# Attention stage of a three-part kernel: another order of the steps within a turn

## What is computed

```python
# q, k, v: 4 x 8 x 576 x 64; mean over 4 neighbouring positions gives q_d, k_d, v_d (144 positions)
out_d = sm_attn(q_d, k_d, v_d)                 # pooled branch: softmax over all 144
out_up = np.repeat(out_d, factor, axis=2)
mask = np.abs(pos[:, None] - pos[None, :]) < factor
scores = np.where(mask, scale * np.matmul(q, k.transpose(0, 1, 3, 2)), -1000000000.0)
out_local = np.matmul(softmax(scores), v)      # local branch: 7 neighbours
x = (out_up + out_local)                       # -> 2304 x 512
h = x @ w_in; x = (h * np.tanh(softplus(h))) @ w_out            # 512 -> 2048 -> 512
...                                            # second block: 512 -> 1024 -> 512
```

## Time and profile before

| | us |
|---|---|
| median of 3 runs (707.36 to 709.15) | 707.73 |
| the profiled execution | 707.11 |
| its span, first to last instruction | 705.3 |
| TensorE busy | 678.3 (96%) |
| VectorE busy | 369.9 (52%) |
| ScalarE busy | 262.5 (37%) |
| GpSimd busy | 183.2 (26%) |

### The profile page before, as it was taken

One profiled execution on the slowest core, in us unless ns is written; L12 is line 12 of the kernel. 1 busy time (PEld: TensorE's weight loads), 2 busy tenths in 40 slices (PEclk: granted clock), 3 DMA queues, 4 the chain that ended last, 5 costly groups with the idle time before them and its releaser, 6 DMA issues.

```text
span 705.3 us, 12609 instructions
## 1 busy us (share of the span) xinstructions
PE 678.3 (96%) x5098; PEld 626.7 (89%) x5098; DVE 369.9 (52%) x675; ACT 262.5 (37%) x583; POOL 183.2 (26%) x220
## 2 busy tenths in 40 slices
PE   5878799999999999999999999999999999999998
PEld 5667689999999999999999999999778888888886
DVE  8999966642223222322232332664796667756671
ACT  5788874321112111211121112136564444535441
POOL 5989820000000000000000000574535434354100
PEclk9999999999999999999999999999999999999999
DMA  7887783000000000000000030002000000000001
GB/s 239 234 236 221 209 309 147 1 1 0 1 1 1 1 0 1 1 1 1 0 2 1 1 119 1 1 1 90 31 16 16 30 31 16 16 31 30 31 16 45
DMA packets 25657, 37.51 MB, mean 53 GB/s; under 512 B 2944, under 2 KB 13184, under 8 KB 25472
## 3 DMA queue, kind: packets, MB, share of 16 engines
q1 hardware_dynamic: 25600, 36.72, 16.3%
HBM read 31.99 MB, written 4.72 MB: 52 GB/s over the span
## 4 chain that ended last, share of the span: by engine, by line
PE 82%; DVE 10%; issue 3%; ACT 2%; POOL 2%; DMA 1%; SPq 0%; DVEq 0%; ACTq 0%; POOLq 0%
PE psum L685 28%; PE psum L671 28%; PE psum L778 12%; PE psum L755 11%; PE psum L764 2%; DVE prob L1110 2%; DVE mx L1107 1%; DVE xy L1134 1%; ACT pprob L839 1%; DVE den L1124 1%; DVE psum L1098 1%; POOL ylo L548 1%; DMA qkT<-kT_dram 1%; DVE so L1296 1%; DVE kd L1073 1%
## 5 line engine op out<-in xcount | busy, mean ns | idle before, releaser
L1193 DVE CAST ghi<-g_sb 128x384 fp32r<-128x384 f32 x96 | 39.6, 413 | 245.5 <-PE psum L685 188.8
L894 ACT ACTIVATE g_sb<-psum 128x384 f32<-128x384 f32 x96 | 47.0, 490 | 292.6 <-PE psum L671 288.3
L671 PE MATMUL psum<-xhi,whi 128*128 128x384 f32 x384 | 129.7, 338 | 1.3 <-ACT g_sb L894 0.7
L671 PE MATMUL psum<-xlo,whi 128*128 128x384 f32 x384 | 129.1, 336 | 0.0
L685 PE MATMUL psum<-ghi,whi 128*128 128x384 f32 x384 | 129.1, 336 | 0.0
L685 PE MATMUL psum<-ghi,wlo 128*128 128x384 f32 x384 | 129.1, 336 | 0.0
L671 PE MATMUL psum<-xhi,wlo 128*128 128x384 f32 x384 | 129.1, 336 | 0.0
L685 PE MATMUL psum<-glo,whi 128*128 128x384 f32 x384 | 129.1, 336 | 0.0
L520 POOL TENSOR_TENSOR t<-raw 128x1024 f32<-128x1024 f32 x1 | 2.6, 2609 | 350.3 <-PE psum L685 350.3
L671 PEld LDWEIGHTS psum<-xhi,whi 128*128 128x128 f32 x384 | 72.3, 188 | 2.4 <-ACT g_sb L894 1.2
L685 PEld LDWEIGHTS psum<-glo,whi 128*128 128x128 f32 x384 | 72.3, 188 | 0.1
(11 more groups left out here) (123 smaller groups left out, 1052.2 us busy)
## 6 DMA issues: line engine op xcount, KB each, us to landing
wraw<-w_dram SPq DMA_DIRECT2D x12, 512.0 KB, 8.1
qkT<-qT_dram SPq DMA_DIRECT2D x16, 288.0 KB, 3.7
qkT<-kT_dram SPq DMA_DIRECT2D x16, 288.0 KB, 5.1
out_dram<-ob SPq DMA_DIRECT2D x18, 256.0 KB, 2.0
v<-v_dram SPq DMA_DIRECT2D x16, 256.0 KB
vw<-v_dram SPq DMA_DIRECT2D x32, 128.0 KB, 3.2
wraw<-w_dram SPq DMA_DIRECT2D x16, 256.0 KB, 6.3
raw<-w_dram SPq DMA_DIRECT2D x1, 2048.0 KB, 7.2
```

Of the source, the lines that this page charges most:

```text
L671: ins = nc.tensor.matmul(bank, a[:, w], b[:, kdx, :], start=(kdx == 0 and n == 0), stop=(kdx == KD - 1 and n == 2))
L894: nc.scalar.activation(g_sb[:, f % HR, :], psum[:, HB1 + f % HB, 0:N1], ACT.Mish).then_inc(g_ok, 1)
L1193: nc.vector.tensor_copy(ghi[:, f % GR, :], g_sb[:, f % HR, :]).then_inc(ghi_ok, 1)
```

## The change

Three orders are changed; no instruction is added or taken out. TensorE makes the pooled scores of a turn ahead of the local ones. ScalarE makes the pooled exponentials right after the scaling of the unit before, ahead of `evict_pooled` and `exp_local` (and, in turn 15, ahead of `split_x` and `weights_in_high(1)`). VectorE takes the pooled maxima first, then `subtract_local`, then `evict_local` of unit u - 2, then the keys of the next unit, then the extras, and `sum_local` and `denominators` last. In turn 15 (`UNITS - 1`) the eviction stays behind the denominators.

```diff
                 if u < UNITS:
+                    score_pooled(u)
                     score_local(u)
-                    score_pooled(u)
...
                     normalise_pooled(u - 1)
+                if u < UNITS:
+                    exp_pooled(u)
                 if u == UNITS - 1:
                     split_x(0, KD - 1)
                     weights_in_high(1)
@@ -906,7 +908,6 @@
                     evict_pooled(u - LATE)
                 if u < UNITS:
                     exp_local(u)
-                    exp_pooled(u)
...
                 if u < UNITS:
+                    maxima_pooled(u)
                     subtract_local(u)
-                    maxima_pooled(u)
-
-                    if u in ADDED:
-                        add_pooled(0, ADDED.index(u))
-                    if u - 1 in ADDED:
-                        split_x(0, ADDED.index(u - 1))
-                    if u == UNITS - 1:
-                        split_x(0, KD - 1)
-                    sum_local(u)
-                if u == UNITS - 1:
-                    denominators(u)
+
+
+                if LATE <= u != UNITS - 1:
+                    evict_local(u - LATE)
                 if u < UNITS - 1:
                     if u % 2 == 0:
                         pool_keys(u + 1)
+                if u in ADDED:
+                    add_pooled(0, ADDED.index(u))
+                if u - 1 in ADDED:
+                    split_x(0, ADDED.index(u - 1))
+                if u == UNITS - 1:
+                    split_x(0, KD - 1)
+                if u < UNITS:
+                    sum_local(u)
                     denominators(u)
-                if u >= LATE:
+                if u == UNITS - 1:
                     evict_local(u - LATE)
```

## The result

The changed kernel takes 712.76 us (median of 6 runs, 712.24 to 713.99) against 708.43 for the kernel before on the same chip (6 runs, 707.14 to 710.14): a ratio of 1.0066 (95% interval 1.0052 to 1.008). It is slower, as forecast, but by 4.3 us and not by 2.5, and outside the range of 706.9 to 712.2. The profiled execution took 712.9 us with a span of 711.1; before it was 707.11 and 705.3. So +5.8 us of span have to be found. Of the runs further down, one of the five of evict15 took 2752.59 us and is left out of its median and ratio.

The account below looks back on a forecast made before the run. The attention part was bound by GpSimd's work of two turns plus 0.39 us waiting around L1124, 10.06 us a pair. Start 2.25, first pair 0.44, extras -1.35 and end 1.2 gave +2.5: 710.2 us, range 706.9 to 712.2.

Parts of the forecast that it names:

- the end: Turns 14 and 15: `exp_local(15)` queued behind ScalarE's casts delays L1126, and `hidden(0, 1)` equally; -0.1 or +1.2, taken as +1.2.
- Queues passed: Steady turns: `evict_pooled` now behind `exp_pooled`, next turn's transposes waiting for it by `od_ok`; no slack, no loss.
- slow TensorE at the start: Turn 1: TensorE's groups may stay slow as the first ones are, costing 0 to 0.4 us; taken as 0.
- first pair: First two ticks: L1124 of turn 2 no longer slips in ahead of L498; +0.44 us, bounds 0 and 0.44.
- The start itself: Turn 0: local scores now follow pooled scores, which need the pooled keys, so the first L1126 comes 2.25 us later.
- Plain pairs: Steady pairs of turns without extras: L1124 still waits for GpSimd, ticks stay 10.06 us apart, price 0.
- Extras pairs: Three pairs with add and split: keys move ahead of the split, next tick 0.45 us earlier, -1.35 in all.
- rival 1: Turn 14: VectorE keeps the port instead of GpSimd; 1.25 us less, 708.9; chance 0.2.
- Rival 2: Steady pairs: L1124 slips in ahead of L498, seven pairs take 9.67 instead of 10.06; 707.0; chance 0.13.
- Rival 3: Even turns: the moved eviction waits for the values, 0.3 us lost in each of seven pairs; 712.3; chance 0.15.
- Rival 4: Start: costs less because TensorE's slow groups shorten or overlap; 709.0 at best; chance 0.07.

Follow-up runs that it names:

- evict15: The changed kernel with ScalarE's `evict_pooled(13)` ahead of `exp_pooled(15)` in turn 15: 711.12 us, ratio 1.0037.
- act15: The changed kernel with ScalarE's old order in turn 15 alone: 709.42 us, ratio 1.0022.
- warm14: The changed kernel with 14 extra matmuls on TensorE just before the transposes of turn 16: 713.26 us, ratio 1.0072.
- noeps: The changed kernel without the small addition of 1e-9 to the denominators: 713.31 us, ratio 1.0078.
- turn0: The changed kernel with the old order of all three engines in turn 0 alone: 711.65 us, ratio 1.0046.
- ends: The changed kernel, old order in turns 0 and 1, on ScalarE in turn 15, and for VectorE's eviction in turn 14: 707.04 us, ratio 0.999.
- turn01_we: The changed kernel with the old order in turns 0 and 1, and the first quarter of the weights loaded earlier: 711.58 us, ratio 1.0057.
- bnoeps: The kernel before without the small addition of 1e-9 to the denominators: 707.37 us, ratio 0.999.
- after_we: The changed kernel with the first quarter of the weights loaded in turns 4, 6, 8 and 10: 713.71 us, ratio 1.0082.
- turn01: The changed kernel with the old order of all three engines in turns 0 and 1: 710.69 us, ratio 1.004.

## Why the prediction was wrong, and where it was right

**The step that failed: the end.** I put `exp_local(15)` behind `exp_pooled(15)`, the split and the weight cast, and then said that `hidden(0, 1)` "moves by the same amount" as L1126. Behind the same three things stands `evict_pooled(13)`, and behind that, by `od_ok`, the transposes of turn 16 and all of TensorE's work. I had written this dependence down for the steady turns ("Queues passed") and not followed it into turn 15, where ScalarE has the extra casts. It cost 1.21 by itself and 1.63 more through TensorE's clock; evict15 and act15 both bring it back to 2.18 us. The first part of that step was right in kind: the way from tick 14 to the reciprocal grew by 0.64 and not 1.2. 0.26 of the difference is ScalarE's lengths, which I added, while neighbours start 0.10 to 0.12 before the one ahead ends (0.51 long, 0.40 to the next); 0.19 is that turn 15 began 1.91 after the tick and not 2.1.

**Mis-sized: slow TensorE at the start.** I had bounded it by 0 and 0.4 and took 0. In turn 1 of after eight matmuls of the pooled scores take 1.23, in turn 2 the usual 0.71 (TensorE in order of time):

```profile
11.90 1.23 PE L587 MATMUL psum<-kd,qd 64*64 64x144 f32 x8 [2.52 <-DVE kd L1074]
...
16.68 0.71 PE L587 MATMUL psum<-kd,qd 64*64 64x144 f32 x8 [0.45 <-POOL qd L488]
```

It is the 0.43 by which the first pair exceeds its +0.44: in warm14, with the same order, these eight happened to take 0.71, and its first pair took 10.07. The granted clock reads 1.00 over the slow ones in after (11.85 to 13.10), so the record does not say why they were slow. Of the start's extra 0.70, 0.54 are the first load, which landed later in this profile (first pooled queries at 4.79, 4.25 before; 4.18 to 4.94 in all profiles), so that is scatter. The start itself was +2.41, forecast +2.25.

**Right.** Plain pairs (forecast 10.06, measured 10.06, 10.06 and 10.14), with the wait for GpSimd as their cause (the three runs without the addition). Extras pairs -0.45 forecast, -0.51 to -0.54 measured, 10.90 to 10.94 for "11.0". GpSimd gets the port in turn 14, so rival 1 falls. GpSimd and VectorE of after there:

```profile
86.83 1.44 POOL L505 TENSOR_TENSOR prob<-prob,rden 128x640 f32<-128x640 f32 x1 [0.46 <-DVE rden L1127]
...
86.66 0.49 DVE L1150 TENSOR_TENSOR xy<-xy,od 128x384 f32<-128x384 f32 x1
87.07 1.74 DVE L1160 TENSOR_TENSOR wlo<-wraw,whi 128x512 fp32r<-128x512 f32 x1
```

The weight split takes 0.68 where it does not wait (before, at 86.11). Here it takes 1.74, from 87.07 to 88.81, and ends 0.54 after L505 (88.27), just as at 94.36 it ends 0.54 after the L505 of turn 15. The Trainium skill (SBUF — State Buffer, "Who interferes with whom") lets an operation that has begun keep the port; these rows agree, as the add came first and is 0.49 long, while L505, which came second, took 1.44 and not 1.26.

**Rivals.** Rival 2 (L1124 slips ahead) did not occur in a plain pair. Rival 3, the eviction waiting for values, has its mechanism but another place: not every even turn, but in after turn 14 alone, by 0.39 us, and up to 3.52 in noeps; its 712.3 is near the measured time by chance, not by its cause. Rival 4 fell: the start cost more.

## What to carry over

When a step is moved ahead on an in-order engine, list every instruction that it is moved past in the first and the last turns too, and for each ask who waits; a steady state that comes out to 0.1 us says nothing about the ends, where undoing the new order in three places here gave back more than the whole loss. A gap opened in front of TensorE can cost twice, the idle time and the slow matmuls behind it (here 1.6 to 2.8 us more). And a faster loop asks its loads earlier: before counting a gain per turn, check that the last turns' data can be there.

## What the runs showed of the hardware

- Behind 3.61 us without work TensorE's granted clock was 0.56 over 93.3 to 97.2, and twelve matmuls took 3.84 us and not 2.26; behind 3.50 us in turn0 it was 0.50 from the first transposes on. Behind 0.94 us (act15), 1.22 (ends) and 1.43 (noeps) there was no such loss, but behind 1.45 us in warm14 the clock was 0.62: the length of the gap alone does not tell. The Trainium skill (TensorE: Matmul & The Clock Gate, "HAM oscillation — how this bites in real kernels") warns that waits between groups of matmuls make the next group start slow; the traces agree, by 1.63 us for the gap in after and 2.79 for that in turn0 (7.48 against 4.69).
- A unit's values can land so late that the eviction waits, 0.39 us in after and up to 3.69 in turn01_we. Of ten such waits of over 1 us in all profiles, seven end about 10 to 12.5 us behind the issue of a load of weights; the other three (bnoeps, 74.64; after_we, 74.02; turn01_we, 86.90) do not.
- The reciprocal of 13 columns takes 0.24 us also while GpSimd is at work (noeps: 38.19, with L497 from 37.57 to 38.84), while the addition to the same 13 columns took up to 1.00 (turn01, at 14.04). So it is not any small operation that waits for GpSimd.

What stays open: why warm14's added matmuls began 1.45 us late, why the same gap costs 1.63 us in after and 2.79 in turn0, what makes the values late, and what a load order made for the faster loop would be worth.
